# Feed-forward tiles of 384 tokens in place of 288, with layer-two scratch and outputs sharing places in X

## The reference

```
h = x @ w_in                        # 512 -> 2048
x1 = (h * np.cos(h)) @ w_out        # 2048 -> 512
rms = np.sqrt(np.mean(x1 * x1, axis=-1, keepdims=True) + 1e-06)
xn = x1 / rms * rms_g
g, val = xn @ w_gate, xn @ w_val    # 512 -> 1536 each
out = (g / (1 + np.exp(-g)) * val) @ w_out2   # 1536 -> 512
```

## Time and profile before

| | us |
|---|---|
| median of 3 executions | 1266.7 (1266.56 to 1267.24) |
| span of the profiled execution | 1264.6 |
| median less that span (what lies around the instructions) | 2.1 |
| PE busy | 1219.2 (96% of the span) |
| DVE busy | 725.5 (57%) |
| ACT busy | 526.9 (42%) |
| POOL busy | 497.8 (39%) |
| mean granted clock of TensorE | 0.995 of full speed |

### The profile page before, as it was taken

How to read it: one execution, slowest core, us unless ns; L and a number is a source line. 1 busy time by engine, 2 the same in 40 slices (tenths; PEclk the granted TensorE clock), 3 DMA queues, 4 the chain that set the end, 5 groups by cost and what they waited for, 6 DMA issues and landing times. The chain is left out here.

```text
span 1264.6 us, 26124 instructions
## 1 busy us (share of the span) xinstructions
PE 1219.2 (96%) x9106; PEld 1096.9 (87%) x9106; DVE 725.5 (57%) x1764; ACT 526.9 (42%) x1188; POOL 497.8 (39%) x588
## 2 busy tenths in 40 slices
PE   6789999999979999999999999999999999999998
PEld 2266777777669999999999999999999999999998
DVE  8977777777779777878778788552112020211111
ACT  6977777777723434344444433212212121212111
POOL 3056666666666424344243444551111111111111
PEclk9989999999999999999999999999999999999999
DMA  5844425252135000000000002340000000000000
GB/s 183 248 146 136 141 95 160 92 179 66 64 95 147 2 1 0 0 0 1 0 0 0 0 0 67 92 117 20 1 19 19 0 19 0 19 0 19 0 19 19
DMA packets 47590, 69.06 MB, mean 55 GB/s; under 512 B 3744, under 2 KB 28480, under 8 KB 47552
## 3 DMA queue, kind: packets, MB, share of 16 engines
q1 hardware_dynamic: 47552, 68.60, 17.4%
HBM read 53.25 MB, written 15.34 MB: 54 GB/s over the span
## 5 line engine op out<-in xcount | busy, mean ns | idle before, releaser
L817 PE MATMUL banks<-x_high,w_high_rest 128*128 128x288 f32 x992 | 293.3, 296 | 0.5 <-PEq L1010 0.5
L818 PE MATMUL banks<-x_low,w_high_rest 128*128 128x288 f32 x992 | 292.8, 295 | 0.0
L819 PE MATMUL banks<-x_high,w_low_rest 128*128 128x288 f32 x992 | 291.8, 294 | 0.0
L1372 DVE TENSOR_TENSOR product<-angle_or_silu,banks 128x288 f32<-128x288 f32 x96 | 43.4, 452 | 312.2 <-PE banks L819 312.2
L1391 POOL TENSOR_TENSOR product_low<-product,product_high 128x288 fp32r<-128x288 f32 x96 | 77.6, 808 | 356.4 <-ACT product_high L1332 356.4
L1190 POOL TENSOR_TENSOR product_low<-product,product_high 128x288 fp32r<-128x288 f32 x128 | 110.4, 863 | 242.5 <-ACT product_high L1070 242.5
L817 PE MATMUL bank<-product_high,w_high_rest 128*128 128x288 f32 x672 | 201.3, 300 | 3.5 <-POOL product_low L1391 2.0
L819 PE MATMUL bank<-product_high,w_low_rest 128*128 128x288 f32 x672 | 197.8, 294 | 0.0
L818 PE MATMUL bank<-product_low,w_high_rest 128*128 128x288 f32 x672 | 197.7, 294 | 0.0
L819 PEld LDWEIGHTS banks<-x_high,w_low_rest 128*128 128x128 f32 x992 | 186.7, 188 | 0.0
L817 PEld LDWEIGHTS banks<-x_high,w_high_rest 128*128 128x128 f32 x992 | 185.9, 187 | 0.7 <-issue 0.7
(11 more groups left out here) (97 smaller groups left out, 2539.4 us busy)
## 6 DMA issues: line engine op xcount, KB each, us to landing
raw_qk<-in_qk SPq DMA_DIRECT2D x32, 576.0 KB, 3.7
bias_scratch<-bias_stage SPq DMA_DIRECT2D x36, 288.0 KB, 3.1
bias<-bias_scratch SPq DMA_DIRECT2D x32, 288.0 KB, 3.1
w_raw<-in_w_out SPq DMA_DIRECT2D x28, 256.0 KB, 2.6
values<-in_v SPq DMA_DIRECT2D x16, 320.0 KB, 4.0
w_raw<-in_w_in SPq DMA_DIRECT2D x16, 256.0 KB, 2.9
out_t<-X SPq DMA_DIRECT2D x7, 576.0 KB, 3.0
w_raw<-in_w_gate SPq DMA_DIRECT2D x12, 256.0 KB, 3.0
```

The source lines that it names most:

```text
L817: nc.tensor.matmul(out, high, x_high, start=start, stop=False)
L818: nc.tensor.matmul(out, high, x_low, start=False, stop=False)
L819: return nc.tensor.matmul(out, low, x_high, start=False, stop=stop)
L1372: dve.tensor_tensor(s[:, :], silu[:, :], val_ps[f % 2][:, 0:NT], ALU.mult).then_inc(s_ready, 1)
```

## The change: what it does

- `NT` goes from 288 to 384, so `TILES_T` from 8 to 6. All elementwise instructions and matmuls of the two feed-forward layers are 384 columns wide. A bank of PSUM holds 512.
- The norm works on sub-tiles of 128 tokens and not 96 (still three a tile). `make_diag` on DVE, the matrix of ones and `diag` go; `spread` becomes three transposes of the norm factor, read as a column that is repeated 128 times, through an identity matrix. It waits for POOL's power directly.
- Memory: `silu`, the gated product and the gated layer's squares are put in tile 0's place in `X`, whose contents are used up by then, and outputs of tile t go to the place of tile t+1 (the last one's to place 0).
- The gated layer's weights start again at slot 0 of the weight store and not at slot 32; four further slots (the "tail") are taken when the cosine layer's buffers are gone. So the 8 units that are split ahead overwrite units of the cosine layer, and POOL waits for PE's `down` before each of them.

```diff
-NT = 288
+NT = 384
-SUB = 96
+SUB = P
@@ Weights
     def part(self, low, w):
-        slot = w % self.SLOTS
-        return self.head[low][:, slot, :] if slot < HEAD else self.rest[low][:, slot - HEAD, :]
+        slot = w if w < U1 else w - U1
+        if slot < HEAD:
+            return self.head[low][:, slot, :]
+        return self.rest[low][:, slot - HEAD, :] if slot < U1 else self.tail[low][:, slot - U1, :]
@@ Norm
-    def make_diag(self, dve, t):
-        dve.wait_ge(self.inv_rms_ready, t + 1)
-        for i in range(NSUB):
-            dve.tensor_scalar(self.diag[:, i, :], self.sub_ident[:, :], self.inv_rms[:, i:i + 1], None, ALU.mult
-                              ).then_inc(self.diag_ready, 1)
-
     def spread(self, pe, t):
-        pe.wait_ge(self.diag_ready, (t + 1) * NSUB)
-        self.nc.tensor.matmul(self.rms_ps[:, 0:NT], self.ones[:, :], self.diag[:, :, :].rearrange("p a b -> p (a b)"),
-                              start=True, stop=True).then_inc(self.spread_ready, 1)
+        pe.wait_ge(self.inv_rms_ready, t + 1)
+        for i in range(NSUB):
+            last = self.nc.tensor.transpose(self.rms_ps[:, i * SUB:(i + 1) * SUB],
+                                            self.inv_rms[:, i:i + 1].broadcast_to([SUB, P]), self.ident[:, :])
+        last.then_inc(self.spread_ready, 1)
@@ Chunks
-        self.inner = sb(ctx, "angle_or_silu", [P, NT], F32)
-        self.product = sb(ctx, "product", [P, NT], F32)
+        X3 = self.features.X3
+        self.silu, self.gated = X3[:, 0, 0:NT], X3[:, 1, 0:NT]
@@ cos_layer_phase, GpSimd, the units split ahead
-                        if w == weights.SLOTS:
-                            pool.wait_ge(down_done, t * DOWNS + 2)
+                        pool.wait_ge(down_done, t * DOWNS + ((w - U1) // 2 + 1))
                         weights.split_high(pool, w)
@@ gated_layer_phase
+    norm.squares = [X3[:, k, 0:NT] for k in (2, 3)]
-                             X3[:, parts, bass.ds(t * NT, NT)]).then_inc(out_stored, 16)
+                             X3[:, parts, bass.ds(home * NT, NT)]).then_inc(out_stored, 16)
             with sp.Fori(0, T - 1) as t:
-                store(t, slice(0, KC))
-            store(T - 1, slice(0, KC - 1))
-            store(T - 1, slice(KC - 1, KC))
+                store(t, t + 1, slice(0, KC))
+            store(T - 1, 0, slice(0, KC - 1))
+            store(T - 1, 0, slice(KC - 1, KC))
```

More of the change, by code:

```diff
@@ L738, in __init__ @@
         self.head = [sb(ctx, f"w_{part}_head", [P, HEAD, UNIT], F32R) for part in ("high", "low")]
-        self.rest = None
+        self.rest, self.tail = None, None
         self.raw = sb(ctx, "w_raw", [P, RAW, UNIT], F32)
@@ L745, in add_rest, with add_tail @@
     def add_rest(self, sb, ctx):
-        self.rest = [sb(ctx, f"w_{part}_rest", [P, self.SLOTS - HEAD, UNIT], F32R) for part in ("high", "low")]
+        self.rest = [sb(ctx, f"w_{part}_rest", [P, U1 - HEAD, UNIT], F32R) for part in ("high", "low")]
+    def add_tail(self, sb, ctx):
+        self.tail = [sb(ctx, f"w_{part}_tail", [P, U2 - U1, UNIT], F32R) for part in ("high", "low")]
     def part(self, low, w):
-        slot = w % self.SLOTS
-        return self.head[low][:, slot, :] if slot < HEAD else self.rest[low][:, slot - HEAD, :]
+        slot = w if w < U1 else w - U1
+        if slot < HEAD:
+            return self.head[low][:, slot, :]
+        return self.rest[low][:, slot - HEAD, :] if slot < U1 else self.tail[low][:, slot - U1, :]
     def block(self, low, w, k):
@@ L831, in __init__ @@
         self.X3 = X[:, :].rearrange("p (k t) -> p k t", k=KC)
-        self.squares = [sb(ctx, f"squares{i}", [P, NT], F32) for i in range(2)]
+        self.squares = None
         self.by_dm = sb(ctx, "by_dm", [P, 1], F32)
-        self.ones = sb(ctx, "ones", [SUB, P], F32)
-        self.sub_ident = sb(ctx, "sub_ident", [SUB, SUB], F32)
+        self.ident = sb(ctx, "token_ident", [SUB, SUB], F32)
         self.mean_eps = sb(ctx, "mean_eps", [SUB, NSUB], F32)
@@ L838, in __init__ @@
         self.inv_rms = sb(ctx, "inv_rms", [SUB, NSUB], F32)
-        self.diag = sb(ctx, "diag", [SUB, NSUB, SUB], F32)
         self.rms_g = sb(ctx, "rms_g", [P, KC], F32)
@@ L978, in cos_layer_phase @@
     turns = sb(ctx, "turns", [P, NT], I32)
-    angle, g, gh, gl = chunks.inner, chunks.product, chunks.high, chunks.low
+    angle, g = sb(ctx, "angle", [P, NT], F32), sb(ctx, "g", [P, NT], F32)
+    gh, gl = chunks.high, chunks.low
+    norm.squares = [sb(ctx, f"squares{i}", [P, NT], F32) for i in range(2)]
     h_ps, h_ready = chunks.h_ps, chunks.h_ready
@@ L1110, in _ @@
             act.wait_ge(chunks.gate_ready, 1)
-            act.activation(chunks.inner[:, :], chunks.gate_ps[:, 0:NT], ACT.Silu).then_inc(chunks.silu_ready, 1)
+            act.activation(chunks.silu, chunks.gate_ps[:, 0:NT], ACT.Silu).then_inc(chunks.silu_ready, 1)
         @block.vector
@@ L1217, in cos_layer_phase, with gated_layer_phase @@
     ctx.close()
-def gated_layer_phase(nc, sem_of, norm, features, weights, chunks, out_t):
+def gated_layer_phase(nc, sb, sem_of, norm, features, weights, chunks, out_t):
     ctx = ExitStack()
-    silu, s, sh, sl = chunks.inner, chunks.product, chunks.high, chunks.low
+    weights.add_tail(sb, ctx)
+    silu, s, sh, sl = chunks.silu, chunks.gated, chunks.high, chunks.low
     gate_ps, val_ps = chunks.gate_ps, chunks.val_ps
@@ L1331, in tile @@
                             act.wait_ge(out_ready, t * KC)
[L1332 removed]
+                    act.activation(sh[f % 2][:, :], s, ACT.Copy).then_inc(s_high, 1)
             for d in norm.KEPT_BY_ACT:
@@ L1343, in _, with keep @@
         def _(dve):
-            def keep(t):
+            def keep(t, home):
                 for d in range(KC):
                     dve.wait_ge(out_ready, t * KC + (d + 1))
-                    dve.tensor_copy(X3[:, d, bass.ds(t * NT, NT)], acc[d][:, 0:NT]).then_inc(out_kept, 1)
+                    dve.tensor_copy(X3[:, d, bass.ds(home * NT, NT)], acc[d][:, 0:NT]).then_inc(out_kept, 1)
             def tile(t, first, last):
@@ L1360, in tile @@
                     elif f == 1:
-                        keep(t - 1)
+                        keep(t - 1, t)
                     dve.wait_ge(val_ready, c1)
@@ L1383, in _ @@
             tile(T - 1, False, True)
-            keep(T - 1)
+            keep(T - 1, 0)
         @block.gpsimd
@@ L1433, in build @@
         cos_layer_phase(nc, sb, sem_of, norm, features, weights, chunks)
-        gated_layer_phase(nc, sem_of, norm, features, weights, chunks, out_t)
+        gated_layer_phase(nc, sb, sem_of, norm, features, weights, chunks, out_t)
 def position_tables():
```

26 lines of the change are left out of this document (9 added, 17 removed).

## The result

The changed kernel takes 1233.3 us (median of 4, 1232.4 to 1233.6) against 1267.0 of before in the same session: a ratio of 0.9733, 95% interval 0.9719 to 0.9747. It is faster by 33.6 us. The forecast was 1231.5 us with a span of 1229.5; the profiled span is 1231.8. That execution took 1233.59 us, 1.8 us over its span, where the forecast added 2.1; the same 1.8 us lie over the span in the executions of the kernel before.

What follows compares the result with a forecast made beforehand. PE, in use 96% of the span, was taken as the bound. Matmuls -21.8, excess -14.1 and a later layer start +0.8 gave -35.1 us, so 1231.5 us; 1226 to 1247 by the excess ends, stated range 1224 to 1254.

Steps and rivals of the forecast that it cites:

- The wider matmul: Split matmuls of both layers: 4896 at 173.3 ns (160 plus a fixed 13.3), 848.6 us, 21.8 less than 870.4.
- the proportional cost: Rival: a matmul costs the same per column, 177.8 ns at 384; time 1253 us, chance 0.13.
- the floor: Rival: 13.3 ns is a floor under 288-column matmuls that 384 pass, 160 ns each; time 1178 us, chance 0.07.
- shorter distances in some `down` chunks: Gated layer: every fourth start distance shorter at the same 288 columns, taken as sign for a fixed part per matmul.
- The excess: Time of both layers' stretches beyond their matmuls: from 35.3 to 21.2 us, 14.1 less.
- the gated loop: Gated layer after its first tile: excess from -0.84 to -0.6 us if the short distances stay.
- the first gated tile: Weight-ring chunks 6.1 us, under PE's 6.24; excess from 8.04 to 2.3 us, left for the barrier and first chunk.
- The first cosine tile: Rest of that tile: DVE's turn 4.0 to 4.1 us, under PE's 4.16; excess from 3.63 to 0.8 us.
- The start: Start of the cosine layer: its chain grows with the columns, excess from 5.27 to 5.9 us (5.3 to 7.0).
- `spread` and `means` at nothing: Norm in each tile: three transposes and `means` loading 128 columns counted at nothing; uncovered, transposes 0.33 us a tile.
- Before the layers: End of attention: DVE's four `x_low` (4.51 us) make the layers begin 0.3 to 1.5 us later, 0.8 taken.
- The slower rival: DVE becomes the cosine layer's bound; over 4.53 us in all 96 chunks the gain is gone, 1288 at 4.75; chance 0.03.

Runs made afterwards that it cites:

- experiment 1: A separate kernel of float32r matmuls back to back at eight widths from 128 to 512 columns, then variants and bfloat16; 173.3 ns a matmul at 384 columns.
- experiment 4: The changed kernel with 9 tiles of 256 tokens in place of 384: 1285.6 us, 1.0144 of before.
- experiment 2: The matmul-only kernel with 352, 416, 448, 480 columns and 384 with shifted operand beginnings: 160.0, 188.3, 202.7, 216.7 ns; 173.3 or 176.0 at 384.
- experiment 7: The changed kernel with all four `x_low` of the next tile made ahead of the rough step of chunk 15: 1233.2 us, 0.9740 of before.
- experiment 5: The changed kernel with norm factors spread as before, by DVE's diagonal matrix and PE's product with ones, at 384: 1234.6 us, 0.9748 of before.
- experiment 3: The changed kernel with tiles of 288 tokens and sub-tiles of 96, so without the width: 1264.5 us, 0.9981 of before.
- experiment 8: DVE's copy at the end of attention moved behind the first `x_low`: changed kernel 1227.1 us, with the `x_low` reordering ahead of chunk 15 1228.1, kernel before 1262.1.
- experiment 6: Every DVE clamp done twice: 1259.7 us (0.9945 of before) in the changed kernel at 384, 1300.8 (1.0274) with its tiles at 288.

## Why the prediction was right

- **The wider matmul, 173.3 ns, -21.8 us.** Right to the tenth of a ns, in the kernel and by itself. Experiments 1 and 4 rule out the proportional cost and the floor, which were the two rivals for it. The argument that chose between them was weak, though, and its right end partly luck: I took shorter distances in some `down` chunks as a sign against a plain rate, but irregularities of a few ns turn up at one width by an operand's place alone (experiment 2), and say nothing on how the cost grows with the width.
- **The excess, -14.1 us.** -11.7 measured: right in the main, short by 2.4 us, of which the gated loop is 1.5 and the first gated tile 0.6. The first cosine tile (0.95 for 0.8) came out nearly right in size and not in kind. The forecast had DVE's turn there at 4.0 to 4.1 us, under PE's 4.16; it is 4.24, and DVE still sets the pace. The step that failed is that the two weight splits do not grow: in this tile they went from 0.76 to 0.88 us on the mean (the cause was not looked for). The rest of the working held: the turn grew by a fifth from 3.5 us and PE's chunk by 30%, which is where the 2.7 us came from; experiment 4 shows the same excess grow to 5.5 at the smaller tile. The first gated tile came to 2.86 for 2.3: its middle chunks are 6.24 us, all PE (24.96 us for four). What is left is 1.8 us in its first chunks (the last `product_low` of the cosine layer and the barrier), 0.67 for `means` and 0.33 for the transposes, two pieces that the forecast didn't name there.
- **The start, 5.9.** 6.13, and this is luck. The chain was to grow with the columns; PE's wait for the first `product_low` fell from 1.57 to 1.13 us. The excess is larger because 14 matmuls stand at the lower clock and not 5 as before. The same instructions with 4 have an excess of 4.8 and 5.0 us (experiments 7 and 5), less than the 5.27 of before.
- **The gated loop, -0.6.** The term that was furthest off, by 1.5 us: +0.88. I took it that distances might only fall short of 173.3. In two chunks of each tile, those whose weights lie in the tail, they exceed it, 176.7 ns on the mean (75.04 us a tile for 74.88). Experiment 2 has such a case by the moving operand's place alone; here it would be that of the weights. The kernels of experiments 3 and 4 have the same tail and no such excess at 288 and 256 columns (-1.1 and -0.2 us in their gated loops), so the place alone doesn't make it; the cause is open.
- **`spread` and `means` at nothing.** Right together and not one by one: a tile's transposes cost PE 0.33 us where the product cost 0.49, and `means` rose from 0.53 to 0.67. With the waits at that place `spread` cost 5.4 us in all before and 2.0 now. The 0.33 is the figure that the forecast gave for the case that nothing covers them. Experiment 5 puts the transposes at 1.9 us of gain in six tiles over the product at this width.
- **The last cosine tile, 1.8.** 1.56; PE waits neither for the norm factors nor for the squares. Experiment 3 shows the first of them gone without the width.
- **Before the layers, +0.8.** +0.67. The mechanism was the right one: the four `x_low` went from 4.51 to 4.91 us. Experiment 8 shows that it is worth far more than the term I gave to its growth: the whole wait could go.
- **The sums.** The high ends of the excess terms add up to 34.0, so the forecast's upper end by them is 1244 and not 1247. What lies around the span is 1.8 us and not 2.1. Neither changes the argument.
- **The slower rival, DVE as the bound.** Not met, the turn grew by less than the columns. But experiment 6 shows the edge nearer than the forecast made it: the room is in the plain chunks only, and 0.4 us more a chunk costs 26 us; in the first tile DVE was the bound all along.

## What to carry to other kernels

Read a stream of matmuls by the distance of starts while nothing waits, take the columns off, and what is left is paid once per matmul: here 13.3 ns for float32r, 3.2 us a chunk at 288 columns of which 0.32 is no column. Widening a tile also lengthens each chunk of the bounding engine, and all work that comes once per chunk whatever its width (weight splits, fixed parts of instructions) gets more cover; that was most of the last third of the gain. A room worked out for the usual chunk says nothing of the chunks that carry something more: count the room there, where waits begin.

## What the hardware showed that I had not expected

- The fixed part of a float32r matmul at full clock is 13.3 ns at 256, 320, 352, 384 and 512 columns, 11.7 at 288, 15 at 416, 16 to 20 at 448 and 16.7 at 480. In the kernel it is 13.3 at 288 too. In bfloat16 it is 2.5 at every width measured.
- Float32r matmuls of 128 and of 192 columns both take 111.7 ns with new weights each time; in bfloat16 128 columns take 55.8.
- The same 384 columns take 176.0 ns and not 173.3 if the moving operand begins 32 elements further on, but not 16 or 64.
- An order of two instructions on DVE, ahead of a PE wait of 4.6 us, was worth 6.2 us: 4.4 of the wait, and the rest by a clock that stayed up, 1.0 in the eight matmuls behind the wait and up to 1.0 in the stretch after them.
- After the same wait of 4.6 us the clock stayed low for 14 matmuls in one execution and for 4 in two others, 1.3 us of time.
- Three float32 transposes of 128x128 hold PE for 0.33 us, a float32 product of 384 columns for 0.64, of 288 for 0.49.
